# Order of the two expert products on TensorE: first product in one piece, second product whole

## The chip, the cores and the metric

The kernel runs on one core of a Trainium2 chip. The metric is the device time of one execution in microseconds (us). Its core has TensorE (PE, matmuls), VectorE (DVE), ScalarE (ACT), GpSimd (POOL), and SyncE (SP), which issues DMAs. Each engine works through its own list of instructions in order and waits on semaphores for the others.

## The reference

Three stages follow each other: an attention with a decaying state, and two mixtures of experts. Cut to the part that the change touches:

```python
def _moe_ref(x, expert_emb, tau, w1, w2):          # N = 3072 rows, D = 384, E = 8 experts, F = 1024
    ...
    expert_idx = np.argmax(logits, axis=1)
    ...
    for e in range(E):
        mask = expert_idx == e
        h = np.maximum(x[mask] @ w1[e], 0.0)
        out[mask] = gate_w[mask, None] * (h @ w2[e])

def _moe2_ref(x, w_gate, w_output_gate, w1, w2):   # x is the output of _moe_ref
    logits = x @ w_gate
    e_idx = np.argmax(logits, axis=1)
    ...
    eom = 1.0 / (1.0 + np.exp(-(x @ w_output_gate)))
    ...                                            # the same two products, with weights of its own
        out[mask] = gate_w[mask, None] * eom[mask, e, None] * ye
```

## The kernel before

After the attention the rows are sorted by expert into DRAM, in tiles of 128 rows; a tile belongs to one expert. There are two expert layers, `m = 0` and `m = 1`, and in each a loop over tiles, whose counter is `p`, runs on PE, DVE and ACT at once (27 tiles in the first layer, 28 in the second).

Every product is split in three terms, since x, h and the weights are held as a high and a low part: high times high, high times low, low times high. For a tile PE does:

- `transpose_h(p)` (L1102): eight transposes of `hs`, the hidden activations of tile p. ACT copies them from PSUM as `hT_hi` (L565), and DVE makes the rest, `hT_lo` (L875).
- `first_product(p + 1, n, ...)` (L1087, L1092): nine matmuls of 512 columns for one half n of the hidden columns of the next tile. Six read `xT_hi`, three `xT_lo`. ACT turns the result into `hs` (L560).
- the second product of tile p: 16 matmuls of 384 columns that read `hT_hi` (L1113, `second_product_hi`), and 8 that read `hT_lo` (L1121, `second_product_lo`), all into bank 2. DVE scales the sum into `ybuf` (L894, `gated`).
- `transpose_x(p + 2)` (L1076): three transposes of the tile that a DMA has brought into `xin`.

In the first layer the router of the second layer is worked in as well, on the tile whose output is just finished: `transpose_y` (L1047) transposes `ybuf`; ACT copies it to `yT` (L532); `logits_y` (L1054) multiplies it with the gates' weights; DVE picks the expert as a one-hot row (`choose`, up to L832); `ranks_y` (L1059, L1060) counts the rows ahead of each row; DVE works out the row's place (`place_row`), and GpSimd scatters the row.

Weights arrive as raw pieces, six for an expert. ACT copies each to `w_hi` (`split_hi`, L506) and DVE takes the rest, `w_lo` (`split_lo`, L735). `with_next_expert` does this in two stops of three pieces each: `SOON` in the tile that is the first of an expert, `LATE` in the tile after it, for the expert that comes next. On ACT both stand between the copies of `hT_hi` and the copy of `yT`.

The tile's weights lie in one of two slots. `weights(g)` (L1070, L1071) loads the slot and the number of the expert into registers of PE's sequencer from a table in SBUF.

Of the kernel before, what the change touches and what calls it, by code (L numbers as in the profile page):

```python
# [18 lines left out]
DM = H * D  # L19
# [8 lines left out]
JC = F // P  # L28
# [11 lines left out]
W2 = KC * F  # L40
# [22 lines left out]
def build(nc, rk_in, w_in, rkv_src, seq_in, uflat_in, emb_in, tau_in, wall1_in, wg2_in, wall2_in, out):  # L63
# [4 lines left out]
    with ExitStack() as ctx:  # L68
# [6 lines left out]
        bank = [ctx.enter_context(nc.psum_tensor(f"bank{i}", [P, 512], F32)) for i in range(8)]  # L75
# [87 lines left out]
        w_hi = sb("w_hi", [P, RING, WCOLS], F32R)  # L163
# [773 lines left out]
        def _(pe):  # L937
# [119 lines left out]
            def ranks_y(g, totals=False):  # L1057
                pe.wait_ge(r2["oh"], g)
                pe.matmul(bank[3][:, 32:32 + E], before[:, :], ohr, start=True, stop=False)  # L1059
                last = pe.matmul(bank[3][:, 32:32 + E], ones[:, :], acc, start=False, stop=True)  # L1060
                if totals:
                    pe.matmul(bank[3][:, 48:48 + E], ones[:, :], ohr, start=True, stop=False)
                    last = pe.matmul(bank[3][:, 48:48 + E], ones[:, :], acc, start=False, stop=True)
                last.then_inc(r2["cnt"], 1)

            for m in range(2):
# [35 lines left out]
                            last = pe.transpose(bank[4 + hf][:, j * P:(j + 1) * P], hs[:, n0:n0 + P], ident[:, :])  # L1102
                        last.then_inc(mo["hT_ps"], 1)

                def second_product_hi(g, slot, pieces):

                    pe.wait_ge(w_split, pieces + RAWS)
                    pe.wait_ge(mo["y_sb"], g + 1)
                    for j in range(JC):
                        if j % 4 == 0:  # L1110
                            pe.wait_ge(mo["hT_hi"], 2 * g + j // 4 + 1)
                        for w in (w_hi, w_lo):
                            pe.matmul(bank[2][:, 0:DM], hT_hi[:, j, :],  # L1113
                                      w[:, bass.ds(slot, 1), W2 + j * DM:W2 + (j + 1) * DM].rearrange("p o n -> p (o n)"),
                                      start=(j == 0 and w is w_hi), stop=False)

                def second_product_lo(g, slot):
                    for j in range(JC):
                        if j % 4 == 0:
                            pe.wait_ge(mo["hT_lo"], 2 * g + j // 4 + 1)  # L1120
                        last = pe.matmul(bank[2][:, 0:DM], hT_lo[:, j, :],  # L1121
                                         w_hi[:, bass.ds(slot, 1), W2 + j * DM:W2 + (j + 1) * DM].rearrange("p o n -> p (o n)"),
                                         start=False, stop=(j == JC - 1))
                    last.then_inc(mo["mm2"], 1)

                pe.sem_inc(mo["mm2"], 2)
# [8 lines left out]
                with pe.Fori(0, last) as p:  # L1135
                    slot, pieces = weights(p + 1)
                    transpose_h(p)
                    first_product(p + 1, 0, slot, pieces)
                    if m == 0:
                        transpose_y(p + 1)  # L1140
                    old_slot, old_pieces = weights(p)
                    second_product_hi(p, old_slot, old_pieces)
                    if m == 0:
                        logits_y(p + 1)
                    first_product(p + 1, 1, slot, pieces)
                    transpose_x(p + 2)
                    if m == 0:
                        ranks_y(p + 1)
                    second_product_lo(p, old_slot)

                transpose_h(last)
                slot, pieces = weights(last)
                if m == 0:
                    transpose_y(last + 1)
                    logits_y(last + 1)
                second_product_hi(last, slot, pieces)
                if m == 0:
                    ranks_y(last + 1)
                second_product_lo(last, slot)
                if m == 0:  # L1160
                    transpose_y(last + 2)
                    logits_y(last + 2)
# [46 lines left out]
```

## Time and profile before

| | |
|---|---|
| time, median of 3 runs | 946.95 us (946.66 to 947.95) |
| time of the profiled execution | 947.32 us |
| its span from first to last instruction | 945.6 us |
| PE busy | 775.7 us, 82% of the span |
| DVE busy | 569.5 us, 60% |
| ACT busy | 392.2 us, 41% |
| first expert layer's loop | about 335 to 640 us of the span |
| second expert layer's loop | about 669 to 934 us of the span |

The profile follows one execution. Busy time is the time in which an engine had an instruction of its own in work; PE's matmuls overlap, so that the start of one to the start of the next is their pace, not their duration.

### The profile page before, as it was taken

The numbers are of one execution on the slowest core, as the hardware profiler recorded it, in microseconds if no ns is written. First come the engines' busy times: TensorE is split into PE (matmuls) and PEld (weight loads), VectorE is DVE, ScalarE is ACT, GpSimd is POOL, SyncE is SP. The second block draws the span as 40 slices with busy tenths as digits, with TensorE's granted clock in tenths as the row PEclk, the third lists the DMA queues.
The fourth block names the chain that finished last, engine by engine and source line by source line (L and its number), as shares of the span: only waits on it lengthen the run. The fifth ranks groups of instructions, "written<-read, shape, count | busy, mean of one in ns | idle before, by whom it ended". The sixth has DMA issues, their size and how long they took to land.

```text
span 945.6 us, 20223 instructions
## 1 busy us (share of the span) xinstructions
PE 775.7 (82%) x4774; PEld 678.1 (72%) x4775; DVE 569.5 (60%) x1437; ACT 392.2 (41%) x768; POOL 196.1 (21%) x218
## 2 busy tenths in 40 slices
PE   0686877667780199999999999992999999999995
PEld 0575766556530188989888898881899999999994
DVE  4999999999364035574747556654444535434631
ACT  2344344443470034453535545530443534434531
POOL 5544444445005400000100000000001010101010
PEclk9979788897895599999999999996899999999998
DMA  4453534455174302441414335332344424333310
GB/s 110 126 138 113 148 102 138 116 145 209 35 234 169 118 17 68 132 157 50 160 43 160 100 100 165 101 100 86 101 140 142 136 71 167 109 101 104 104 37 30
DMA packets 46726, 108.30 MB, mean 115 GB/s; under 512 B 6601, under 2 KB 25616, under 8 KB 46704
## 3 DMA queue, kind: packets, MB, share of 16 engines
q1 hardware_dynamic: 29632, 67.91, 23.2%
q10 hardware_dynamic: 11952, 25.88, 9.2%
q0 software_dynamic: 5120, 14.26, 4.1%
q8 instruction: 7, 0.11, 0.1%
q14 instruction: 15, 0.12, 0.0%
HBM read 90.60 MB, written 19.01 MB: 116 GB/s over the span
## 4 chain that ended last, share of the span: by engine, by line
PE 63%; DVE 18%; issue 10%; ACT 3%; ACTq 2%; POOL 1%; SPq 1%; DMA 1%; DVEq 0%; POOLq 0%
PE bank L1087 16%; PE bank L1113 15%; PE bank L1121 8%; PE bank L1092 8%; DVE Q L643 6%; PE bank L1102 5%; DVE SF L653 4%; PE bank L1076 2%; PE bank L1054 2%; PE bank L1029 2%; ACT w_hi L506 2%; DVE Kb L657 2%; DVE St L675 1%; DVE Rq L648 1%; PE bank L1012 1%
## 5 line engine op out<-in xcount | busy, mean ns | idle before, releaser
L735 DVE TENSOR_TENSOR w_lo<-raw,w_hi 128x1024 f32 (+1 forms) x96 | 112.1, 1221 | 66.0 <-ACT w_hi L506 66.0
L1113 PE MATMUL bank<-w_hi,hT_hi 128*128 x440 | 150.3, 342 | 1.0 <-ACT hT_hi L565 0.5
L1113 PE MATMUL bank<-w_lo,hT_hi 128*128 x440 | 147.8, 336 | 0.0
L1087 PE MATMUL bank<-w_hi,xT_hi 128*128 x330 | 138.9, 421 | 1.6 <-ACT xT_hi L556 1.6
L1087 PE MATMUL bank<-w_lo,xT_hi 128*128 x330 | 131.9, 400 | 0.0
L560 ACT ACTIVATE hs<-bank 128x512 f32<-128x512 f32 x110 | 65.1, 592 | 114.1 <-PE bank L1092 106.8
L506 ACT ACTIVATE w_hi<-raw 128x1024 f32 (+1 forms) x96 | 94.8, 1049 | 38.6 <-issue 38.6
L1092 PE MATMUL bank<-w_hi,xT_lo 128*128 x330 | 95.2, 397 | 0.0
L565 ACT ACTIVATE hT_hi<-bank 128x512 fp32r<-128x512 f32 x110 | 59.7, 595 | 76.1 <-PE bank L1102 76.1
L1121 PE MATMUL bank<-w_hi,hT_lo 128*128 x440 | 90.9, 348 | 0.0
L414 POOL DMA_INDIRECT sorted<-yrow,slot x28 | 27.2, 972 | 300.8 <-DVE yrow L853 300.8
L951 PE MATMUL bank<-Rq,Kb 64*128 64x128 f32 x384 | 38.5, 358 | 61.4 <-DVE Kb L657 61.4
L1113 PEld LDWEIGHTS bank<-w_hi,hT_hi 128*128 128x128 f32 x440 | 82.6, 188 | 7.3 <-issue 6.1
L869 DVE TENSOR_TENSOR xT_lo<-bank,xT_hi 128x384 fp32r<-128x384 f32 x57 | 31.8, 558 | 92.5 <-ACT xT_hi L556 92.5
L1113 PEld LDWEIGHTS bank<-w_lo,hT_hi 128*128 128x128 f32 x440 | 82.6, 188 | 1.2
L428 POOL DMA_INDIRECT out<-ybuf,toki x28 | 27.2, 972 | 260.8 <-DVE ybuf L894 260.8
L951 PEld LDWEIGHTS bank<-Rq,Kb 64*128 64x128 f32 x384 | 32.7, 253 | 66.9 <-DVE Kb L657 60.2
L1121 PEld LDWEIGHTS bank<-w_hi,hT_lo 128*128 128x128 f32 x440 | 74.8, 189 | 0.0
L1076 PE MATMUL bank<-ident,xin 128*128 128x128 f32 x171 | 28.7, 278 | 56.1 <-DMA xin<-sorted 56.1
L1092 PEld LDWEIGHTS bank<-w_hi,xT_lo 128*128 128x128 f32 x330 | 62.8, 190 | 14.4
L1087 PEld LDWEIGHTS bank<-w_hi,xT_hi 128*128 128x128 f32 x330 | 63.6, 193 | 12.8 <-issue 2.4
L875 DVE TENSOR_TENSOR hT_lo<-bank,hT_hi 128x512 fp32r<-128x512 f32 x110 | 70.9, 686 | 2.9 <-ACT hT_hi L565 1.3
(194 smaller groups left out, 1320.8 us busy)
## 6 DMA issues: line engine op xcount, KB each, us to landing
raw<-wall_in SPq DMA_DIRECT2D x96, 512.0 KB, 3.9
rkv<-rkv_src ACTq DMA_DIRECT2D x24, 576.0 KB, 5.3
xin<-sorted ACTq DMA_DIRECT2D x59, 194.0 KB
rk<-rk_in SPq DMA_DIRECT2D x48, 192.0 KB, 3.7
wb<-w_in SPq DMA_DIRECT2D x48, 96.0 KB, 3.4
sorted<-padrow SPq DMA_DIRECT2D x16, 194.0 KB, 1.9
sorted<-yrow,slot POOLq DMA_INDIRECT x28, 2.6
out<-ybuf,toki POOLq DMA_INDIRECT x28, 2.6
```

The costliest lines, as they stand in the source:

```text
L506: act.activation(w_hi[:, slot, q * RAWC:(q + 1) * RAWC], raw[:, q], ACT.Copy).then_inc(w_his, 1)
L560: act.activation(hs[:, n * 512:n * 512 + 512], bank[n][:, :], ACT.Relu).then_inc(mo["h_sb"], 1)
L565: act.activation(hT_hi[:, 4 * n:4 * n + 4], bank[4 + n][:, :].rearrange("p (k t) -> p k t", k=4), ACT.Copy)\
L643: last = v.tensor_tensor_scan(Q[:, b, a, 1:C + 1], wb[:, par, a, 0:C], wb[:, par, a, 0:C], 1.0, ALU.mult, ALU.bypass)
L735: v.tensor_tensor(w_lo[:, slot, cols], raw[:, q], w_hi[:, slot, cols].bitcast(F32), ALU.subtract).then_inc(w_split, 1)
L875: v.tensor_tensor(hT_lo[:, 4 * n:4 * n + 4], bank[4 + n][:, :].rearrange("p (k t) -> p k t", k=4), hT_hi[:, 4 * n:4 * n + 4].bitcast(F32), ...
L951: last = pe.matmul(bank[2 * (b % 2) + hf][:, a * C:(a + 1) * C], Kb[q, b, a, :], Rq[q, b, a, :], start=True, stop=True, skip_group_check=True)
L1076: last = pe.transpose(bank[6][:, k * P:(k + 1) * P], xin[:, k * P:(k + 1) * P], ident[:, :])
L1087: pe.matmul(bank[n][:, :], xT_hi[:, k, :], w[:, bass.ds(slot, 1), cols].rearrange("p o n -> p (o n)"), start=(k == 0 and w is w_hi), stop= ...
L1092: last = pe.matmul(bank[n][:, :], xT_lo[:, k, :], w_hi[:, bass.ds(slot, 1), k * F + c0:k * F + c0 + 512].rearrange("p o n -> p (o n)"), st ...
L1113: pe.matmul(bank[2][:, 0:DM], hT_hi[:, j, :], w[:, bass.ds(slot, 1), W2 + j * DM:W2 + (j + 1) * DM].rearrange("p o n -> p (o n)"), start=( ...
L1121: last = pe.matmul(bank[2][:, 0:DM], hT_lo[:, j, :], w_hi[:, bass.ds(slot, 1), W2 + j * DM:W2 + (j + 1) * DM].rearrange("p o n -> p (o n)" ...
```

## The change

PE alone gets another order inside the loops of both expert layers, and at their ends. `first_product` for both halves now stands together, ahead of the router's logits and of the second product. The second product is one function: for each of the eight slices j, both terms of `hT_hi` and the term of `hT_lo` follow one another. Its waits for `hT_lo` stand with those for `hT_hi`. `ranks_y` is called in its middle, ahead of slice 4.

```diff
-                def second_product_hi(g, slot, pieces):
+                def second_product(g, slot, pieces, between=None):
 
                     pe.wait_ge(w_split, pieces + RAWS)
                     pe.wait_ge(mo["y_sb"], g + 1)
                     for j in range(JC):
                         if j % 4 == 0:
                             pe.wait_ge(mo["hT_hi"], 2 * g + j // 4 + 1)
-                        for w in (w_hi, w_lo):
-                            pe.matmul(bank[2][:, 0:DM], hT_hi[:, j, :],
...
-                def second_product_lo(g, slot):
-                    for j in range(JC):
-                        if j % 4 == 0:
                             pe.wait_ge(mo["hT_lo"], 2 * g + j // 4 + 1)
...
+                        if j == 4 and between is not None:
+                            between()
+                        for x, w in ((hT_hi, w_hi), (hT_hi, w_lo), (hT_lo, w_hi)):
+                            last = pe.matmul(bank[2][:, 0:DM], x[:, j, :],
+                                             w[:, bass.ds(slot, 1), W2 + j * DM:W2 + (j + 1) * DM].rearrange("p o n -> p (o n)"),
+                                             start=(j == 0 and x is hT_hi and w is w_hi), stop=(j == JC - 1 and x is hT_lo))
                     last.then_inc(mo["mm2"], 1)
...
                     if m == 0:
                         transpose_y(p + 1)
                     old_slot, old_pieces = weights(p)
-                    second_product_hi(p, old_slot, old_pieces)
+                    first_product(p + 1, 1, slot, pieces)
                     if m == 0:
                         logits_y(p + 1)
-                    first_product(p + 1, 1, slot, pieces)
                     transpose_x(p + 2)
-                    if m == 0:
-                        ranks_y(p + 1)
-                    second_product_lo(p, old_slot)
+                    second_product(p, old_slot, old_pieces, (lambda: ranks_y(p + 1)) if m == 0 else None)
```

The first place is PE in the first layer's loop, behind the loads of `weights(p)`. ISA rows are register steps of the sequencer. Before:

```order
L1047 MATMUL bank<-ident,ybuf 128x128 x3
L1070 ISA
L1070 TENSOR_LOAD tab
L1070 ISA x2
L1071 ISA
L1071 TENSOR_LOAD tab
L1071 ISA x2
L1107 ISA
L1113 ISA
L1113 MATMUL bank<-w_hi,hT_hi 128x384
```

Now, from the last of these loads on:

```order
L1071 TENSOR_LOAD tab
L1071 ISA x2
L1087 ISA
L1087 MATMUL bank<-w_hi,xT_hi 128x512
L1087 REGISTER_ALU
L1087 MATMUL bank<-w_lo,xT_hi 128x512
```

The first product's second half has taken the place of the 16 matmuls of `second_product_hi`; the register step at L1107, which belongs to a wait of the second product, has gone from here.

The second place is PE around the logits (L1054) in the same loop. Before, the 16 matmuls of L1113 stood ahead of them:

```order
L1113 MATMUL bank<-w_lo,hT_hi 128x384
L1054 MATMUL bank<-rtW,yT 128x16 x3
L1087 ISA
L1087 MATMUL bank<-w_hi,xT_hi 128x512
L1087 REGISTER_ALU
```

Now the first product's second half, 9 matmuls, stands ahead of them, and the second product starts behind the transposes of x:

```order
L1092 MATMUL bank<-w_hi,xT_lo 128x512 x3
L1054 MATMUL bank<-rtW,yT 128x16 x3
L1074 ISA
L1076 MATMUL bank<-ident,xin 128x128 x3
L1107 ISA
L1116 ISA
L1116 MATMUL bank<-w_hi,hT_hi 128x384
```

The third place is PE around the ranks (L1059, L1060) and the end of the tile. Before:

```order
L1076 MATMUL bank<-ident,xin 128x128 x3
L1059 MATMUL bank<-r,before 128x8
L1060 MATMUL bank<-r,ones 128x8
L1121 MATMUL bank<-w_hi,hT_lo 128x384 x8
L1135 REGISTER_ALU
L1135 COMPARE_AND_BRANCH
L1099 ISA
```

Now, of the four slices that follow the ranks, the first:

```order
L1116 MATMUL bank<-w_hi,hT_lo 128x384
L1059 MATMUL bank<-r,before 128x8
L1060 MATMUL bank<-r,ones 128x8
L1116 ISA
L1116 MATMUL bank<-w_hi,hT_hi 128x384
L1116 REGISTER_ALU
L1116 MATMUL bank<-w_lo,hT_hi 128x384
L1116 MATMUL bank<-w_hi,hT_lo 128x384
```

Eight matmuls without a register step between the ranks and the loop's branch have become four slices of three matmuls with two register steps each.

## Rows read from the trace of the kernel before

**Rows 1.** Busy time by stretch: span, each engine, PEclk, DMA share, GB/s.

```profile
338.00:640.00 302.00, 297.06 (x1745) 266.32 (x1743) 181.03 (x660) 143.32 (x307) 25.26 (x26) 1.00 0.33 105
672.00:930.00 258.00, 257.10 (x1424) 233.84 (x1424) 121.50 (x204) 111.53 (x177) 25.27 (x26) 1.00 0.34 111
```

**Rows 2.** Waits of PE over the span: us in total, times, longest us.

```profile
PE bank L1054 <- ACT yT L532: 4.7, 9, 1.4
```

**Rows 3.** Groups by line, ACT, 338 to 642 us: busy, mean ns, idle before.

```profile
L506 ACT ACTIVATE w_hi<-raw 128x1024 f32 x42 | 41.4, 1050 | 19.4 <-issue 19.4
```

**Rows 4.** Timeline of PE, a plain tile of layer one: start us, duration us.

```profile
482.31 1.03 PE L1102 MATMUL bank<-ident,hs 128*128 128x128 f32 x8
...
485.27 0.49 PE L1047 MATMUL bank<-ident,ybuf 128*128 128x128 f32 x3
...
485.71 0.43 PE L1113 MATMUL bank<-w_hi,hT_hi 128*128 x1
...
488.59 0.73 PE L1054 MATMUL bank<-rtW,yT 128*128 128x16 f32 x6
...
489.18 0.48 PE L1087 MATMUL bank<-w_hi,xT_hi 128*128 x1
...
491.33 0.49 PE L1076 MATMUL bank<-ident,xin 128*128 128x128 f32 x3
...
492.02 1.64 PE L1121 MATMUL bank<-w_hi,hT_lo 128*128 x8
...
493.50 0.27 PE L1102 MATMUL bank<-ident,hs 128*128 128x128 f32 x1
```

**Rows 5.** Timeline row of PE's weight loads, then lines of PE's sequencer (first, last start).

```profile
485.70 0.19 PEld L1113 LDWEIGHTS bank<-w_hi,hT_hi 128*128 128x128 f32 x1 [0.19 <-issue]
...
L1107 PEldq FUSED_REGOPS  x1: 42/42/42, 485.4 to 485.4; - x1
...
L1113 PEldq FUSED_REGOPS  x3: 46/51/65, 485.6 to 486.1; - x3
```

**Rows 6.** Timeline of ACT and PE, the first layer-one tile of an expert.

```profile
496.97 2.96 ACT L506 ACTIVATE w_hi<-raw 128x1024 f32 x3 [1.75 <-issue]
499.83 0.47 ACT L532 ACTIVATE yT<-bank 128x384 f32<-128x384 f32 x1
500.35 0.84 PE L1054 MATMUL bank<-rtW,yT 128*128 128x16 f32 x6 [0.41 <-ACT yT L532]
...
505.35 0.27 PE L1102 MATMUL bank<-ident,hs 128*128 128x128 f32 x1
```

**Rows 7.** Timeline of ACT and PE, the tile after that one.

```profile
510.94 0.47 ACT L532 ACTIVATE yT<-bank 128x384 f32<-128x384 f32 x1
511.52 0.78 PE L1054 MATMUL bank<-rtW,yT 128*128 128x16 f32 x6
...
516.50 0.27 PE L1102 MATMUL bank<-ident,hs 128*128 128x128 f32 x1
```

**Rows 8.** DVE's timeline and PE's sequencer, the tile of Rows 6.

```profile
502.56 0.29 DVE L832 TENSOR_SCALAR r<-iota,r 128x8 f32<-128x8 f32 x1
...
L1135 PEldq ALU_OP  x1: 32/32/32, 503.0 to 503.0; - x1
...
L1099 PEldq FUSED_REGOPS  x1: 42/42/42, 504.9 to 504.9; - x1
```

**Rows 9.** Chain that ended last, entry of layer two: start us, duration us.

```profile
657.48 2.38 DMA xin<-sorted
...
661.59 2.92 PE bank L1087 x6
```

**Rows 10.** Timeline of DVE and PE, last tile of layer two.

```profile
929.66 0.69 DVE L875 TENSOR_TENSOR hT_lo<-bank,hT_hi 128x512 fp32r<-128x512 f32 x1
...
929.89 0.44 PE L1113 MATMUL bank<-w_hi,hT_hi 128*128 x1 [0.46 <-ACT hT_hi L565]
```

**Rows 11.** Timeline of PE, last tile of layer one.

```profile
633.95 0.84 PE L1054 MATMUL bank<-rtW,yT 128*128 128x16 f32 x6 [1.40 <-ACT yT L532]
```

More of the change, by code:

```diff
@@ L1111, in second_product_hi @@
                             pe.wait_ge(mo["hT_hi"], 2 * g + j // 4 + 1)
-                        for w in (w_hi, w_lo):
-                            pe.matmul(bank[2][:, 0:DM], hT_hi[:, j, :],
-                                      w[:, bass.ds(slot, 1), W2 + j * DM:W2 + (j + 1) * DM].rearrange("p o n -> p (o n)"),
-                                      start=(j == 0 and w is w_hi), stop=False)
-                def second_product_lo(g, slot):
-                    for j in range(JC):
-                        if j % 4 == 0:
-                            pe.wait_ge(mo["hT_lo"], 2 * g + j // 4 + 1)
-                        last = pe.matmul(bank[2][:, 0:DM], hT_lo[:, j, :],
-                                         w_hi[:, bass.ds(slot, 1), W2 + j * DM:W2 + (j + 1) * DM].rearrange("p o n -> p (o n)"),
-                                         start=False, stop=(j == JC - 1))
+                            pe.wait_ge(mo["hT_lo"], 2 * g + j // 4 + 1)
+                        if j == 4 and between is not None:
[4 more added lines that the diff above has]
+                                             start=(j == 0 and x is hT_hi and w is w_hi), stop=(j == JC - 1 and x is hT_lo))
                     last.then_inc(mo["mm2"], 1)
@@ L1155, in _ @@
                     logits_y(last + 1)
[L1156 to L1159, printed above, removed]
+                second_product(last, slot, pieces, (lambda: ranks_y(last + 1)) if m == 0 else None)
                 if m == 0:
```

## The prediction

> **What bounds the kernel now.** I read the busy time by stretch first. In both expert loops PE is busy nearly throughout: 297.06 of 302 us in the first layer, 257.10 of 258 us in the second, at a granted clock of 1.00 [rows 1]. So both loops go at PE's pace, and there are only two things that an order can change: the time in which PE stands, and nothing else, since the matmuls stay the same in number and size. The second layer leaves 0.9 us of standing in 258; it has nothing to gain. Next I read PE's waits: in the first layer it waits for one thing, the copy of yT by ACT ahead of the logits, 4.7 us in 9 waits [rows 2]. The timeline shows when. A plain tile takes 493.50 - 482.31 = 11.19 us [rows 4], and the logits find yT ready. In the first tile of an expert ACT first splits three pieces of weights, from 496.97 for 2.96 us, and the copy of yT ends at 499.83 + 0.47 = 500.30; the logits start at 500.35, with PE idle, and the tile takes 505.35 - 493.50 = 11.85 us [rows 4, 6]. In the tile after it the next three pieces are split; yT is ready at 511.41, the logits start at 511.52, and the tile takes 11.15 us: there the copy comes just in time [rows 6, 7]. The 42 splits of the first layer are 14 such stops of three [rows 3], 7 of each kind, in 26 tiles of the loop; 12 tiles are plain.
>
> A smaller loss stands behind the transposes of y: PE's weight load is idle for 0.19 us because the sequencer only then gets through the register loads and the waits of the second product [rows 5].
>
> **The change, part by part.** Offsets are from a tile's first transpose of h.
>
> *The logits are reached earlier.* Between the transposes of y and the logits stood 16 matmuls, 488.59 - 485.71 = 2.88 us. Now 9 matmuls of the first product stand there, 491.33 - 489.18 = 2.15 us [rows 4]. So PE is at the logits 0.73 us earlier, while nothing on ACT's way to yT has moved: transposes of h, two copies, the splits, the copy. In a plain tile that is harmless. In a tile with splits PE cannot go past the logits, and what was covered is now a wait. Behind the logits there now stands 2.88 us of work instead of 2.15.
>
> First tile of an expert: the logits stay at 500.35, and the 5.00 us from there to the next tile [rows 6] become 5.73. Cost 0.73 us, 7 times: 5.1 us.
>
> The tile after it: the logits could start 0.05 us behind yT, as in the other tile, so at 511.46 instead of 511.52; from there 4.98 us [rows 7] become 5.71. Cost 0.67 us, 7 times: 4.7 us.
>
> *The transposes of y are followed by the first product.* The register step of the second product's waits at 485.4 and the first of its matmuls' register steps at 485.6 lie 0.2 us apart, and then the matmuls start, at 485.71 [rows 4, 5]. The first product's second half has none of these waits, so the sequencer is there 0.2 us sooner and the gap of 0.19 us should all but close. In the 14 tiles with splits this gains nothing, since they are held by yT. In the 12 plain tiles I take 0.17 us: -2.0 us; bounds 0 and -0.19 x 12 = -2.3.
>
> *The ranks stand in the middle.* PE's sequencer stops at the ranks until DVE has the one-hot row, at 502.85 in the tile shown. From there it needs 0.15 us to the branch at 503.0, with the ranks and all eight low terms dispatched on the way, and 1.9 us more for the branch and the next tile's register loads, to 504.9; the next tile's transposes start at 505.35 [rows 4, 6, 8]. That leaves 0.45 us. In the new order four slices with two register steps each stand between ranks and branch. Such slices follow each other by 0.25 us [rows 5], so 1.0 us is added, while the tile's end moves by only 0.73. What is left is 0.18 us, and from the register step at L1107 to the matmul it took 0.3 [rows 4, 5]. So the transposes come late by about 0.1 us in each of the 14 tiles: +1.5 us. Bounds: 0, and 0.3 x 14 = +4.2. In plain tiles the one-hot row is early with the logits, and nothing is late.
>
> *The low parts are wanted earlier.* In the loop DVE has made hT_lo long before: the second product now starts after the whole first product. The cover is missing only in the last tile of the second layer, where there is no first product: PE started at 929.89, behind ACT's copy; the first half of hT_lo is there only at 929.66 + 0.69 = 930.35 [rows 10]. If PE follows 0.05 us behind, as at the logits, the cost is 0.5 us; 0.2 us more for a longer hand-over would make it 0.7. I take 0.6 us, once. In the last tile of the first layer the wait for yT, 1.40 us, covers it [rows 11].
>
> *The transposes of x move some 3 us forward,* ahead of the second product. The transfer takes 2.38 us [rows 9] and is issued by ACT before its first copy of the tile, so it lands by about 3 us into the tile, and the transposes come no sooner than at 5. Hidden. The relu of the second half, the copies of xT and DVE's place_row come earlier too; all of them were covered.
>
> *The pace of the merged product.* The 16 high terms take 0.18 us each with their start, 8 low terms 493.50 - 492.02 = 1.48 us, 0.185 each with theirs [rows 4]. The starts are as many as before. I take the same pace; 0.002 us either way on 440 low terms is 1 us.
>
> **Sum:** 5.1 + 4.7 - 2.0 + 1.5 + 0.6 = +9.9 us. Against the profiled execution, 947.32 us, that is 957.2; the median of the runs is 0.37 us lower, so 956.9. Forecast: 957 us, 1.1% more.
>
> **The rivals.**
>
> *Faster.* The gap behind the transposes of y closes in all 26 tiles and the logits wait no longer than before: -0.19 x 26 + 0.6 = -4.3 us, 942.6 against the median. It decides if ACT has yT within 5.4 us of the tile's start in the tiles with splits as well. The rows have it at 6.80 and 6.06 [rows 4, 6, 7], and nothing on ACT is moved. 3 in 100.
>
> *No change.* The merged product, three terms of one slice in a row, runs at a quicker pace: 0.165 us instead of 0.174 on 1320 matmuls would be -12 us, and the total about 945 to 947. High and low terms keep the same pace now, whatever reads what [rows 4]. 4 in 100.
>
> *The sequencer is late in every tile.* If the four slices behind the ranks cost their 1.0 us also where I count room, 0.3 us in the 12 plain tiles and 0.5 in the 14: +3.6 + 7 on 9.8 + 0.6, about 968. The room in a plain tile speaks against it. 6 in 100.
>
> *The clock falls.* The waits for yT grow from 0.6 to about 1.3 us and double in number. If after each of the 14 PE ran one second product at the lower level, 1.2 GHz, at which six matmuls of the first product took 2.92 us [rows 9], against 0.23 us each now, that is some 4 us each: +56 us, 1013. Against it: a wait of 1.40 us stands in the stretch whose granted clock is 1.00, the 2.4 GHz level [rows 1, 11]. 3 in 100.
> The Trainium skill has a rule for this, "TensorE: Matmul & The Clock Gate", section "A second HAM failure mode: psum-queue depth-cycling": frequent short idle times between groups of matmuls can make the clock swing between its two levels. By that rule the sum would be the 1013 us of this rival; by the trace it stays at 957.
>
> **How the numbers follow.** The forecast's mechanism has the remaining 84 in 100. Its own range: without the sequencer's loss, with the whole gap gained and a quicker pace, 957.0 - 1.5 - 0.3 - 1 = 954.2; with the sequencer's upper bound, half the gap gained and a slower pace, 957.0 + 2.7 + 1 + 1 = 961.7. I give 953.5 to 961.5. A measurement of this kernel tells about 0.2%, 1.9 us, from no change. Faster: 0.03. Within it: 0.04. Slower: 0.93.
>
> **What would show it.** PE's wait for yT at the logits should grow from 4.7 us in 9 waits to about 14 us in 16. The first tile of an expert should take about 12.6 to 12.7 us, the next 11.9, a plain one 11.0, and a tile of the second layer should keep its pace. The idle 0.19 us of the weight load behind the transposes of y should vanish. In the last tile PE should wait for hT_lo. The forecast is wrong if yT is ready earlier in the tiles with splits, if a plain tile grows (the sequencer), or if the granted clock in the loops leaves 1.00.

## The result, and the profile after

The changed kernel takes 961.88 us (median of 4 runs, 961.0 to 963.24), the kernel before 946.86 us beside it (4 runs). The ratio is 1.0157, 95% interval 1.014 to 1.0175: slower, as forecast, and 0.4 us above the upper end of the range. The profiled execution took 963.24 us, 15.92 more than that of before; its span, 961.5 us, is longer by the same 15.9.

I read PE's waits first, over the span: what PE waited for, us in total, times, longest.

```profile
PE bank L1054 <- ACT yT L532: 15.4, 16, 1.4
...
PE bank L1116 <- DVE hT_lo L875: 1.2, 1, 1.2
```

The wait for yT went from 4.7 us in 9 [rows 2] to 15.4 in 16, and in the last tile the low parts are waited for: both were forecast. What was not forecast is in the busy time by stretch. Columns as in [rows 1]; the first two rows are the loops, the other six divide one first tile of an expert, 404.61 to 418.70. The last three figures are the granted clock, the DMA share and GB/s.

```profile
338.00:640.00 302.00, 288.57 (x1665) 261.19 (x1664) 174.49 (x619) 136.85 (x297) 24.29 (x25) 0.97 0.32 104
690.00:940.00 250.00, 249.93 (x1388) 227.26 (x1388) 118.23 (x199) 107.56 (x174) 25.27 (x26) 1.00 0.35 114
404.60:407.00 2.40, 2.40 (x16) 2.12 (x15) 1.91 (x5) 1.09 (x2) 0.97 (x1) 1.00 0.22 83
407.00:409.90 2.90, 2.90 (x16) 2.23 (x14) 0.66 (x2) 1.81 (x2) 0.00 (x0) 1.00 0.00 0
409.90:412.40 2.50, 1.19 (x10) 0.93 (x9) 2.50 (x3) 2.41 (x5) 0.00 (x0) 1.00 0.29 84
412.40:414.00 1.60, 1.60 (x9) 1.60 (x8) 1.46 (x7) 0.00 (x0) 0.00 (x0) 0.63 0.87 310
414.00:416.00 2.00, 2.00 (x8) 2.00 (x7) 0.35 (x4) 1.35 (x5) 0.00 (x0) 0.50 0.87 291
416.00:418.60 2.60, 2.60 (x17) 2.60 (x17) 1.55 (x9) 0.00 (x0) 0.00 (x0) 0.95 0.51 187
```

The granted clock of the first loop is 0.97, where it was 1.00 [rows 1]. Inside the tile it is 1.00 up to 412.40, falls to 0.50 (1.2 GHz, the lower of its two levels) behind a stretch in which PE was busy for 1.19 of 2.50 us, and is back before the tile ends. The second loop keeps 1.00.

The timeline of PE shows what each kind of tile became. First the end of a first tile of an expert that kept its clock, then the tile after it, then a plain tile (start us, duration us, idle before):

```profile
376.09 0.84 PE L1054 MATMUL bank<-rtW,yT 128*128 128x16 f32 x6 [1.30 <-ACT yT L532]
...
381.62 0.34 PE L1116 MATMUL bank<-w_hi,hT_lo 128*128 x1
381.80 0.61 PE L1102 MATMUL bank<-ident,hs 128*128 128x128 f32 x4
...
387.93 0.84 PE L1054 MATMUL bank<-rtW,yT 128*128 128x16 f32 x6 [0.61 <-ACT yT L532]
...
393.65 1.04 PE L1102 MATMUL bank<-ident,hs 128*128 128x128 f32 x8
...
396.61 0.49 PE L1047 MATMUL bank<-ident,ybuf 128*128 128x128 f32 x3
396.85 0.48 PE L1087 MATMUL bank<-w_hi,xT_hi 128*128 x1
...
399.01 0.73 PE L1054 MATMUL bank<-rtW,yT 128*128 128x16 f32 x6
```

Behind the first tile's last matmul at 381.62 the next transposes start 0.18 us later: the sequencer isn't late. The tile after it runs from 381.80 to 393.65, 11.85 us, with a wait of 0.61 us for yT. The plain tile ends at 404.61, where the next fence begins, after 10.96 us; the first product follows the transposes of y with no gap, and the logits find yT ready. Now the tile of the windows above:

```profile
404.61 1.04 PE L1102 MATMUL bank<-ident,hs 128*128 128x128 f32 x8
...
409.29 0.86 PE L1092 MATMUL bank<-w_hi,xT_lo 128*128 x3
411.47 0.84 PE L1054 MATMUL bank<-rtW,yT 128*128 128x16 f32 x6 [1.31 <-ACT yT L532]
412.16 0.52 PE L1076 MATMUL bank<-ident,xin 128*128 128x128 f32 x3
412.44 0.42 PE L1116 MATMUL bank<-w_hi,hT_hi 128*128 x1
...
412.88 0.52 PE L1116 MATMUL bank<-w_hi,hT_lo 128*128 x1
413.20 0.52 PE L1116 MATMUL bank<-w_hi,hT_hi 128*128 x1
...
416.96 0.34 PE L1116 MATMUL bank<-w_hi,hT_lo 128*128 x1
...
418.70 0.27 PE L1102 MATMUL bank<-ident,hs 128*128 128x128 f32 x1
```

The wait is the same, 1.31 us, and yT is as early. But from 412.88 on ten matmuls start 0.32 us apart instead of 0.17, and the tile takes 14.09 us. That is 10 x 0.15 = 1.5 us lost in a single tile.

The lengths of all tiles, worked out from the starts of the first transpose of h (L1102):

```
us per tile               before          after
12 plain tiles            11.20 (mean)    10.99
7 first of an expert      11.87           12.58 in two; 14.08 to 14.14 in five
7 after them              11.20           11.84
second layer, usual       9.58            9.53 (up to 9.93 in four)
last tile to the end      17.21           17.92
```

The first loop is 310.44 instead of 295.93 us long: 7 x 0.71 = 5.0 and 7 x 0.64 = 4.5 for the waits, 5 x 1.52 = 7.6 for the clock, 12 x -0.21 = -2.5 for the plain tiles; together 14.6 (14.5 by the loop's own length, the rest is rounding). The second loop takes 0.8 us less, the tail 0.7 more, the stretch between the loops 0.15 more. The 1.4 us by which the first loop starts later (336.12, before 334.76) belong to no edit: over the kernels below, which have the same work ahead of it, that start lies anywhere from 331.5 to 337.9. The five parts add up to the 15.9 us. The other three runs of the changed kernel left no trace, so in how many of their tiles the clock fell isn't known.

### The profile page after: what moved, and what is told of

Same layout as the page of the kernel before. It is cut to its first block, busy times and chain, and to the rows that moved or that the text cites. A ratio compares the mean times of both kernels' runs of the same rounds, so it can differ in the third digit from the quotient of the medians.

```text
span 961.5 us, 20305 instructions
## 1 busy us (share of the span) xinstructions
PE 773.9 (80%) x4774; PEld 679.3 (71%) x4775; DVE 568.1 (59%) x1437; ACT 388.3 (40%) x768; POOL 197.3 (21%) x218
## 4 chain that ended last, share of the span: by engine, by line
PE 57%; DVE 16%; issue 10%; ACT 4%; POOL 4%; ACTq 3%; DMA 2%; SPq 1%; DVEq 0%; POOLq 0%
PE bank L1116 25%; PE bank L1087 12%; PE bank L1092 6%; DVE Q L643 5%; PE bank L1102 4%; DVE SF L653 3%; ACT w_hi L506 2%; PE bank L1076 2%; PE bank L1054 2%; POOL sorted L403 2%; PE bank L1029 2%; DVE Kb L657 2%; ACTq L239 1%; DMA xin<-sorted 1%; PE bank L1012 1%
## 5 line engine op out<-in xcount | busy, mean ns | idle before, releaser
L1116 PE MATMUL bank<-w_hi,hT_hi 128*128 x440 | 158.4, 360 | 1.2 <-DVE hT_lo L875 1.2
L1116 PE MATMUL bank<-w_lo,hT_hi 128*128 x440 | 151.9, 345 | 0.0
L1116 PE MATMUL bank<-w_hi,hT_lo 128*128 x440 | 151.7, 345 | 0.0
L1116 PEld LDWEIGHTS bank<-w_hi,hT_hi 128*128 128x128 f32 x440 | 85.4, 194 | 1.7 <-issue 1.4
L1116 PEld LDWEIGHTS bank<-w_hi,hT_lo 128*128 128x128 f32 x440 | 85.6, 195 | 0.0
L1116 PEld LDWEIGHTS bank<-w_lo,hT_hi 128*128 128x128 f32 x440 | 85.5, 194 | 0.0
L560 ACT ACTIVATE hs<-bank 128x512 f32<-128x512 f32 x110 | 63.0, 586 | 50.1 <-PE bank L1092 50.1
L1087 PEld LDWEIGHTS bank<-w_lo,xT_hi 128*128 128x128 f32 x330 | 63.5, 192 | 11.1
```

The costliest lines, as they stand in the source:

```text
L560: act.activation(hs[:, n * 512:n * 512 + 512], bank[n][:, :], ACT.Relu).then_inc(mo["h_sb"], 1)
L1087: pe.matmul(bank[n][:, :], xT_hi[:, k, :], w[:, bass.ds(slot, 1), cols].rearrange("p o n -> p (o n)"), start=(k == 0 and w is w_hi), stop= ...
L1116: last = pe.matmul(bank[2][:, 0:DM], x[:, j, :], w[:, bass.ds(slot, 1), W2 + j * DM:W2 + (j + 1) * DM].rearrange("p o n -> p (o n)"), star ...
```

## The experiments

**The order alone.** The kernel before, with the next tile's second half of the first product moved; the three terms of the second product stay apart.

```diff
-                    second_product_hi(p, old_slot, old_pieces)
+                    first_product(p + 1, 1, slot, pieces)
                     if m == 0:
                         logits_y(p + 1)
-                    first_product(p + 1, 1, slot, pieces)
                     transpose_x(p + 2)
+                    second_product_hi(p, old_slot, old_pieces)
                     if m == 0:
                         ranks_y(p + 1)
                     second_product_lo(p, old_slot)
```

> The kernel before with only the first product's second half moved ahead of the logits and of the high terms; high and low terms stay apart, with the ranks between them. Theory: the early logits alone make the wait for yT and the fall of the granted clock, so the time is about that of the changed kernel, 960 to 963 us; the first tile of an expert takes 12.6 us, or 14.1 where the clock falls. Rival, that the merged product or the ranks in its middle bring the fall: 952 to 955 us, no tile of 14.1 us.

It took 962.0 us (one run; 946.34 before). Tile by tile it is the changed kernel: 10.99, 12.57, 11.83 us, and 14.07 to 14.14 in the same five first tiles of an expert. One of those on PE's timeline:

```profile
410.84 0.84 PE L1054 MATMUL bank<-rtW,yT 128*128 128x16 f32 x6 [1.29 <-ACT yT L532]
...
412.24 0.51 PE L1113 MATMUL bank<-w_hi,hT_hi 128*128 x1
412.54 0.53 PE L1113 MATMUL bank<-w_lo,hT_hi 128*128 x1
```

A tile of the second layer takes 9.53 us, as in the changed kernel. So, as far as one run tells, the whole effect is the order's, the 0.05 us gained in the second layer too. Merging the terms and placing the ranks in their middle cost nothing here.

**The merging alone.** The second product with its three terms together, in its old place: five slices, logits, first product, transposes of x, ranks, three slices.

```diff
-                    second_product_hi(p, old_slot, old_pieces)
+                    second_product(p, old_slot, old_pieces, rng=range(0, 5))
...
-                    second_product_lo(p, old_slot)
+                    second_product(p, old_slot, old_pieces, rng=range(5, JC))
```

> The kernel before with the three terms merged but in the old place: slices 0 to 4 of the second product (15 matmuls) ahead of the logits, then the first product's second half, the transposes of x, the ranks, and slices 5 to 7. Theory: the logits find yT as before, no fall of the clock, so within 2 us of the kernel before; if the register steps behind the ranks hold the sequencer, the first tile of an expert is 0.3 us longer, 2 us in all. Rival, that merging costs by itself: 953 us or more.

955.22 us (953.48 to 958.78), ratio 1.0105, interval 1.0076 to 1.0134. I had expected no more than 2 us; the time is where the rival of the expectation had it. The clock is 1.00, so the loss is another one. Three slices are 9 matmuls where 8 stood; that is 0.17 us behind the wait. And the sequencer is late. The register step ahead of the transposes, by line and engine (first and last start), for the end of a first tile of an expert:

```profile
L1099 PEldq FUSED_REGOPS  x1: 42/42/42, 416.0 to 416.0; - x1
```

And the same place on PE's timeline:

```profile
415.86 0.34 PE L1119 MATMUL bank<-w_hi,hT_lo 128*128 x1
416.14 0.65 PE L1102 MATMUL bank<-ident,hs 128*128 128x128 f32 x4
```

The step comes at 416.0, behind the last matmul's start, and the transposes start 0.28 us behind that matmul instead of 0.17. First tiles of an expert take 12.28 to 12.40 us, those after them 11.62 to 11.80, plain ones 11.22 in the mean (before: 11.20). In the tiles after them 0.13 of the 0.52 us lost lies ahead of the logits, which start 6.40 us into the tile instead of 6.27 (means), and 0.39 behind them, 5.32 instead of 4.93: the ninth matmul's 0.17, and in the tile that ends at 427.89 another 0.16 between the last matmul and the transposes (0.33 us instead of 0.17). The late sequencer that I had feared for the changed kernel is real, but shows where PE waits less for yT.

**The transposes of x ahead of the logits**, in the changed kernel. PE then stands 0.3 us less in a tile with splits.

```diff
                     first_product(p + 1, 1, slot, pieces)
+                    transpose_x(p + 2)
                     if m == 0:
                         logits_y(p + 1)
-                    transpose_x(p + 2)
```

> The changed kernel with the transposes of x ahead of the logits instead of behind them. The wait for yT is 0.33 us shorter in 14 tiles: -4.6 us. Theory that the length of the wait in which PE stands decides on the clock: from 1.4 to 1.1 us standing, fewer or no falls, down to 950 us. Rival, that the whole stretch without long matmuls decides, 2.5 us before and 2.2 now: falls stay, 955 to 958 us.

958.01 us (957.85 to 958.94), ratio 1.013, interval 1.0113 to 1.0146. The clock falls in no tile of the loop. The busy time of the first loop:

```profile
338.00:640.00 302.00, 290.86 (x1706) 260.51 (x1705) 176.34 (x638) 138.09 (x301) 24.93 (x26) 1.00 0.32 104
```

And a first tile of an expert on PE's timeline:

```profile
410.17 0.84 PE L1054 MATMUL bank<-rtW,yT 128*128 128x16 f32 x6 [1.00 <-ACT yT L532]
...
415.42 0.34 PE L1116 MATMUL bank<-w_hi,hT_lo 128*128 x1
415.84 1.09 PE L1102 MATMUL bank<-ident,hs 128*128 128x128 f32 x8
```

The wait is 1.00 us instead of 1.30 and the clock stays. But the tile shortens only to 12.53, not to 12.28: 0.42 us pass between the last matmul and the transposes, a quarter of a microsecond more than its pace. Here the sequencer is the bound, as the step of the forecast on the ranks had it. The tiles after them take 11.87 to 12.12: longer than in the changed kernel, since ACT's splits begin 0.30 us later in them (3.05 us into the tile). Why they do isn't shown.

**PE kept busy while it would stand.** The changed kernel with eight matmuls of 384 columns to an unused place ahead of the logits, in every tile of the first layer. What they compute is read by nothing.

```diff
+                        for k in range(8):
+                            pe.matmul(bank[3][:, 128:512], xT_hi[:, k % 3, :],
+                                      w_hi[:, bass.ds(slot, 1), (k % 3) * F:(k % 3) * F + 384].rearrange("p o n -> p (o n)"),
+                                      start=True, stop=True, skip_group_check=True)
                         logits_y(p + 1)
```

> The changed kernel with 8 extra matmuls of 384 columns ahead of the logits in the first layer's loop; they go to an unused part of bank 3 and nothing reads them. They fill the wait in the first tile of an expert, 8 x 0.174 = 1.4 us. Theory, that standing makes the clock fall: granted clock 1.00 in the loop, first tile of an expert 12.6 to 12.7 us in all seven; plain tiles and second tiles at about 12.4 us, so the whole at about 975 us. Rival, that the fall has another cause: tiles of 14.1 us remain, 983 us.

975.4 us (one run). All seven first tiles take 12.57 to 12.60 us, all others of the loop 12.37 to 12.58. In the stretch 338 to 640 us:

```profile
338.00:640.00 302.00, 302.00 (x1794) 278.77 (x1793) 167.67 (x595) 131.60 (x283) 23.33 (x24) 1.00 0.30 98
```

With 1.4 us more work in them (PE stood for 1.3) the five fallen tiles are 1.5 us shorter. The fillers are all that was added, so the fall needs PE's standing; the rest of the tile's rows doesn't bring it about by itself.

**How long it must stand.** The same with two such matmuls, 0.33 us: PE waits as long as with the transposes of x first, but these stay behind the logits.

> The changed kernel with two matmuls of 384 columns to an unused place ahead of the logits in every tile of the first layer (they compute nothing that is used), 0.33 us of PE. In the first tile of an expert PE then stands 1.1 us instead of 1.45, as long as in the kernel with the transposes of x ahead of the logits, but the transposes stay behind the logits. Theory that the length of the standing makes the clock fall: no tile falls, the seven first tiles take 12.58, the plain and the others grow by 0.2 to 0.33, the total is 961.9 - 7.6 + 12 x 0.33 + 7 x 0 = about 958. Rival, that the row of short matmuls behind the wait (logits and transposes of x, nine in all) makes it fall: five tiles still take 14.1, the total about 966.

958.19 us (one run; 947.31 before). First tiles 12.55 to 12.58, those after them 11.82 to 11.87, plain ones 11.33. The loop's busy time:

```profile
338.00:640.00 302.00, 293.38 (x1743) 266.32 (x1742) 175.85 (x635) 137.32 (x299) 24.30 (x25) 1.00 0.32 104
```

And one of its waits on PE's timeline:

```profile
410.23 0.84 PE L1054 MATMUL bank<-rtW,yT 128*128 128x16 f32 x6 [0.97 <-ACT yT L532]
```

In the first tiles of an expert a wait of 0.97 us is never followed by a fall here, one of 1.30 us in the changed kernel is in five of seven. The rival, that the short matmuls behind the wait are enough by themselves, is out: they stand here as they did there. (This holds for these tiles. In the last tile of the layer, outside the loop, PE waits 1.41 us, and the clock falls there in this kernel too.) A third of a microsecond of useless work makes the kernel some 4 us faster (958.2 against 961.9, each beside about 947 of before).

**A longer stop in the old order.** The kernel before with the logits ahead of the second half of the high terms, so that PE stands longer than in the changed kernel (`between` is `logits_y`).

```diff
                     for j in range(JC):
                         if j % 4 == 0:
                             pe.wait_ge(mo["hT_hi"], 2 * g + j // 4 + 1)
+                        if j == 4 and between is not None:
+                            between()
```

> The kernel before with the logits ahead of slice 4 of the high terms, so behind 8 of them instead of 16; nothing else is moved. They are reached 1.4 us earlier. Theory that standing makes the clock fall, now without the new order: the first tile of an expert stands for about 2.0 us and its clock falls in most of the 7, 13.3 us + 1.5 us = 14.8 us; the tile after stands for 1.2 us, less than the 1.4 us at which it fell, and takes 12.4 us; plain tiles keep 11.2 us. In all about 975 us. Rival, that the fall belongs to the new order: 965 us, granted clock 1.00.

971.64 us (one run). The clock falls here too, so it needs no new order, and it falls less often than I expected: two of seven first tiles (14.85 and 14.89 us, the others 13.29 to 13.32) and the two tiles behind those (14.13 and 14.12, with waits of 1.21 and 1.24 us; the others 12.56 to 12.59, with 1.04 to 1.14). The profile puts these waits down to `issue`, but the logits start as soon as ACT has copied yT (456.95 + 0.47 = 457.42, logits at 457.52). Two first tiles, the one that kept its clock and the one that didn't:

```profile
409.12 0.81 PE L1054 MATMUL bank<-rtW,yT 128*128 128x16 f32 x6 [1.82 <-issue]
415.54 0.71 PE L1102 MATMUL bank<-ident,hs 128*128 128x128 f32 x5
...
457.52 0.81 PE L1054 MATMUL bank<-rtW,yT 128*128 128x16 f32 x6 [1.82 <-issue]
465.48 0.71 PE L1102 MATMUL bank<-ident,hs 128*128 128x128 f32 x5
```

The same wait, 1.82 us, and from the logits to the next tile 6.42 us in one, 7.96 in the other. So the length of the wait alone doesn't say whether the clock falls.

**The logits inside the second product**, ahead of its third slice; the ranks ahead of the seventh. It is meant to give the changed kernel its cover back.

```diff
                     first_product(p + 1, 1, slot, pieces)
                     transpose_x(p + 2)
-                    second_product(p, old_slot, old_pieces, (lambda: ranks_y(p + 1)) if m == 0 else None)
+                    second_product(p, old_slot, old_pieces,
+                                   at={2: lambda: logits_y(p + 1), 6: lambda: ranks_y(p + 1)} if m == 0 else {})
```

> The changed kernel with the logits moved into the second product, ahead of slice 2, and the ranks ahead of slice 6. The logits then come at 6.8 us into a tile, when yT is there: no wait worth naming, clock 1.00. But the sequencer gets from the one-hot row to the next tile's transposes in 0.15 + 0.5 (two slices) + 1.9 us, which is late: plain tiles 11.4 us, first tiles of an expert 12.0, in all 952 to 956 us. Rival, that the sequencer has room: 11.0 and 11.2 us, about 942 us.

953.45 us (one run). No fall; first tiles 12.0 to 12.1, those after them 11.3 to 11.5, plain ones 11.23 to 11.29 (but 11.47 in the loop's first and 11.08 in its last). The waits for yT are gone from PE's list in that loop, and the sequencer's have come in their place. PE's waits, 336 to 630 us:

```profile
PE bank L1102 <- issue: 4.9, 12, 0.6
```

The next transposes wait for nothing that the profile shows but PE's own sequencer. So this place of the logits gives the cover back and loses most of it to the sequencer: 8 us faster than the changed kernel, still some 7 slower than before. Other places at this end weren't tried.

**The register loads moved.** The kernel before, with the loads for the next tile behind the transposes of h, those for the old tile ahead of the transposes of y, in both layers.

```diff
-                    slot, pieces = weights(p + 1)
                     transpose_h(p)
+                    slot, pieces = weights(p + 1)
                     first_product(p + 1, 0, slot, pieces)
+                    old_slot, old_pieces = weights(p)
                     if m == 0:
                         transpose_y(p + 1)
-                    old_slot, old_pieces = weights(p)
```

> The kernel before with the table loads moved on PE alone: those for the next tile behind the transposes of h, those for the old slot ahead of the transposes of y. The gap of 0.2 us behind the transposes of y closes; that helps only the 12 plain tiles, since the others are held by yT: 944.5 us, -2.4 us. Rival, that the loads only shift the gap to another place: no change.

969.88 us (968.43 to 972.72), ratio 1.0238, interval 1.0217 to 1.0259. In the first layer it did what was expected (plain tiles 11.0, the others as before). In the second each tile takes 10.44 us instead of 9.58, 0.86 more on 27 tiles: 23 us. PE's timeline there:

```profile
713.55 1.04 PE L1102 MATMUL bank<-ident,hs 128*128 128x128 f32 x8
714.68 0.49 PE L1087 MATMUL bank<-w_hi,xT_hi 128*128 x1
...
716.16 0.86 PE L1092 MATMUL bank<-w_hi,xT_lo 128*128 x3
717.28 0.44 PE L1113 MATMUL bank<-w_hi,hT_hi 128*128 x1 [0.26 <-issue]
```

From the transposes of h to the first product it takes 1.13 us (in the kernel before 0.80, in the second layer's tile that starts at 736.79), and in front of the second product PE stands again. It is the first load's move that costs this: with the second alone moved, below, the second layer keeps 9.58 us. The sequencer used to do the loads while PE worked off what was queued ahead of the transposes. In this tile the last step of them comes only at 714.3, and the first product starts at 714.68. In the first layer the same loads cost nothing, the first product follows the transposes by 0.79 us: there they begin 1.35 us ahead of the transposes (493.2, 494.55), in the second layer 0.9 us ahead (723.1, 723.99). Why the two layers differ isn't shown further.

**The same, with the logits between the high and the low terms of the first product's second half**, and the ranks ahead of the last four low terms.

> The run with moved table loads, and the logits between the high and the low terms of the first product's second half (behind 22 matmuls and so at about 7.35 us into a tile, past yT's 6.8), the ranks ahead of the last four low terms. No wait for yT, no sequencer late: 11.0 us in all 26 tiles, 936 to 938 us. Rival, that the late ranks make DVE and the sequencer late: 11.3 us or more in tiles with splits, 943 us or more.

978.69 us (977.73 to 980.53), ratio 1.0342, interval 1.032 to 1.0365. Every tile of the first layer but the loop's first takes 11.68 to 11.92, also the plain ones; a tile of the second 10.2. PE's waits, 340 to 640 us:

```profile
PE bank L1087 <- issue: 7.4, 25, 0.4
```

The first product behind the transposes waits for the sequencer in 25 tiles. The moved loads alone don't do that: in the kernel above they cost the first layer nothing (plain tiles 11.0 us). What is new here is the late logits and ranks, as the rival of the expectation had it; by how much each of them counts isn't told. The logits start 8.28 us into the tile at 405.32, not at 7.35. That a tile of the second layer takes 10.2 us and not 10.44, in the same order, isn't explained either.

**Only the second load moved**, from the kernel before.

```diff
                     first_product(p + 1, 0, slot, pieces)
+                    old_slot, old_pieces = weights(p)
                     if m == 0:
                         transpose_y(p + 1)
-                    old_slot, old_pieces = weights(p)
```

> The kernel before with one edit in both layers: the register loads of the old tile's slot and pieces stand ahead of the transposes of y, so the sequencer does them while PE is still busy with the first product; the other loads stay where they are. Theory of the sequencer: the gap of 0.19 us behind the transposes of y closes in the plain tiles, which go from 11.19 to about 11.0 us, nothing changes in the tiles with splits (they are held by yT) or in the second layer; 12 x -0.19 = -2.3, so 944.6 (range 943.5 to 945.8). Rival: the gap belongs to the waits and not to the loads, then 946.9.

945.53 us (10 runs, 943.23 to 947.81; 21 runs of before in the same series, 947.32), ratio 0.9977, interval 0.9962 to 0.9992. The plain tiles take 11.00 us, the second layer 9.58. That is the gap of [rows 5], gained without moving the logits. Either is enough to close it: here the waits of the second product still stand there and the loads are gone, in the changed kernel the loads stand there and the waits are gone.

**And the second layer in the new order**, the first layer in the old.

```diff
+                    if m == 1:
+                        first_product(p + 1, 1, slot, pieces)
+                        transpose_x(p + 2)
                     second_product_hi(p, old_slot, old_pieces)
                     if m == 0:
                         logits_y(p + 1)
-                    first_product(p + 1, 1, slot, pieces)
-                    transpose_x(p + 2)
-                    if m == 0:
+                        first_product(p + 1, 1, slot, pieces)
+                        transpose_x(p + 2)
                         ranks_y(p + 1)
```

> As the run before it, and in the second layer alone the first product stands in one piece ahead of the second (terms apart as before). The clock cannot fall there, since nothing waits for yT. By the traces of the changed order a tile of the second layer goes from 9.58 to about 9.53 us, 24 times, less up to 0.7 us where the transposes of x now wait for their transfer: 943.3 to 944.3. Rival: the pace of the second layer comes from the merging and not from the order, then as the run before it.

943.37 us (10 runs, 942.49 to 945.41), ratio 0.9972, interval 0.9955 to 0.9989. A tile of the second layer takes 9.53 us, save one of 10.34, one of 9.79 and two of 9.58 and 9.62, where the transposes of x come later. These take back nearly all of the 24 x 0.05 = 1.2 us. What the order adds to the kernel above isn't told apart by the ratios.

**And the transposes of x ahead of the logits in the old order.**

```diff
                     if m == 0:
+                        transpose_x(p + 2)
                         logits_y(p + 1)
                         first_product(p + 1, 1, slot, pieces)
-                        transpose_x(p + 2)
                         ranks_y(p + 1)
```

> As the run before it, and in the first layer the transposes of x stand ahead of the logits, so 0.3 us of work lies ahead of the logits and not behind them. Where PE waits for yT the tile should shorten by 0.3 us: 7 first tiles of an expert from 11.87 to about 11.57, 7 tiles after them from 11.20 to about 11.0: -3.3 us, so about 940.5. Rival: the sequencer cannot be back from the one-hot row in less time, 11.75 in the first tiles: 942.5. Rival on the other side: the transposes of x wait for their transfer, which makes it no faster than the run before it.

941.1 us (6 runs, 938.95 to 942.66), ratio 0.9935, interval 0.9912 to 0.9957: the fastest kernel of this study. A first tile of an expert:

```profile
407.64 0.49 PE L1076 MATMUL bank<-ident,xin 128*128 128x128 f32 x3
...
408.44 0.84 PE L1054 MATMUL bank<-rtW,yT 128*128 128x16 f32 x6 [0.32 <-ACT yT L532]
...
413.14 1.03 PE L1102 MATMUL bank<-ident,hs 128*128 128x128 f32 x8
```

From the logits to the next tile it is 4.70 us instead of 5.00 [rows 6], and the tile takes 11.54. It is the reverse of the change in question: more cover ahead of the wait for yT, less work behind it. The 0.9935 is for all three edits together: the second load, the second layer's order and this one.

## Why the prediction was off

**The two waits for yT** were right in place, number and size: 0.71 us in each first tile of an expert against a forecast of 0.73, 0.64 in each tile after it against 0.67. **The gap behind the transposes of y** closed in the plain tiles, 0.21 us each against 0.17. **The pace of the merged product** is unchanged. **The last tile** waits for hT_lo and is 0.71 us longer, against 0.6.

**The step that failed is the last rival, "The clock falls".** I had the waits grow from 0.6 us, while a first tile of an expert showed 0.41 [rows 6]; they grew to 1.3. I gave it 3 in 100, priced it for all 14 tiles or none, at 4 us each, and left it out of the sum because one wait of 1.40 us had gone by at a granted clock of 1.00 [rows 1, 11]. It falls in five of the seven first tiles and costs 1.52 us in each, 7.6 us in all. Without it the changed kernel would stand at 961.9 - 7.6 = 954.3, inside the range (by the profiled execution, the only one whose tiles are known, 963.2 - 7.6 = 955.6). The measurements on which this rests: kept busy, the same tiles don't fall; with 0.33 us less standing they don't either; with the order changed and nothing else they do.

The evidence against it was luck. The wait of [rows 11] is one wait, the only one of its length. The changed kernel has the same wait in the same place, 1.40 us ahead of the logits of the first layer's last tile, and there the clock did fall. First the kernel before, then the changed one, in the same columns as above:

```profile
634.50:637.00 2.50, 2.50 (x17) 2.50 (x17) 1.22 (x8) 0.64 (x4) 0.00 (x0) 1.00 0.01 3
```

```profile
650.00:652.50 2.50, 2.50 (x16) 2.50 (x17) 1.23 (x8) 0.67 (x4) 0.00 (x0) 0.85 0.02 7
652.50:656.00 3.50, 3.50 (x16) 3.50 (x16) 1.05 (x8) 0.00 (x0) 0.00 (x0) 0.62 0.00 0
```

Nor does it take the new order. The kernel with only the second load moved has the kernel before's own last tile, instruction for instruction, with the same wait, and the clock falls in it:

```profile
634.56 0.84 PE L1054 MATMUL bank<-rtW,yT 128*128 128x16 f32 x6 [1.40 <-ACT yT L532]
```

```profile
637.60:640.60 3.00, 3.00 (x15) 3.00 (x14) 0.34 (x4) 0.00 (x0) 0.00 (x0) 0.65 0.00 0
```

Of the 14 traces of this study, that of before among them, eleven have a wait of 1.40 or 1.41 us there, and the clock falls behind it in nine, all but the kernel before and the one with eight fillers. Nothing is seen of these falls in the time: from this tile's start to the second loop's it takes 38.17 us before, 38.19 with the fall shown. Whether a wait of this length is followed by a fall varies, so one that wasn't says little of seven more. The size was wrong as well: I took a whole second product at the lower level, and it was ten of its 24 matmuls.
The Trainium skill, "TensorE: Matmul & The Clock Gate", section "A second HAM failure mode: psum-queue depth-cycling", says that frequent short idle times between groups of matmuls can make the clock swing; on the direction this case's trace agrees (0.97 in the loop, 0.50 inside a tile).

**The sequencer** was put at +1.5 us and cost nothing: behind the ranks the transposes follow at the pace of the matmuls, 0.18 us. It has no room to spare, though. Where PE waits 0.3 us less, or the logits come later, the sequencer ends the tile, and both repairs of the new order, transposes of x first and logits inside, end at 958.0 and 953.5 us. With the transposes of x first, where the sequencer is the bound, it is 3.17 us from the end of the one-hot row (412.67) to the next transposes (415.84). The changed kernel has 3.22 for it (378.58 to 381.80), so 0.05 us to spare. My terms add up to 0.15 + 1.0 + 1.9 + 0.3 = 3.35 us, 0.2 too many.

**The transposes of x are not always hidden.** Four tiles of the second layer are 0.03 to 0.40 us longer, 0.7 us together: PE now reaches the transposes 5.0 us into the tile (7.8 before), and the transfer isn't always there. The longest of the four, by the waits of 723.6 to 733 us and by what the trace has on xin:

```profile
PEld bank L1076 <- DMA xin<-sorted: 0.5, 1, 0.5
```

```profile
DMA to landing us min/median/max: 6.1/6.1/6.1
```

In the round of the loop before it the same transfer took 2.3 us, which I had taken for all. **A tile of the second layer** is otherwise 0.05 us shorter, 1.2 us in all, and the loop's first tile 0.3; I had them unchanged. With the 0.7 us back the second loop is 0.8 us shorter.

**What stays open:** which of the waits of 1.3 us and more are followed by a fall. Five of seven fall after 1.30 us, the same five in two kernels, and two of seven after 1.82. In one last tile of the first layer, that of the kernel with the logits in the first product, it fell behind two waits of 0.74 and 0.94 us. The length of the wait alone doesn't decide it, and the stretch ahead of it (the same matmuls in the tile that fell and in the one that didn't) doesn't either. The DMA traffic doesn't: in the first 1.6 us of the second product its share is 0.87 in the tile that fell (412.40 to 414.00) and 0.87 in one that kept its clock (377.00 to 378.60), and in the fallen last tiles above it is 0.00 to 0.02.

## What to carry to other kernels

When an order moves a wait forward on the engine that is the bound, the loss is the cover taken away, per tile, and it can be read to a few hundredths of a microsecond from two rows; but on TensorE add to it what the clock may take where the wait grows, as here from 1.00 to 1.30 us, and don't rule that out by a single wait that went well: look at the same place in several traces. Ask in the same breath where PE's sequencer stands: its loads, moved to a place with too little queued ahead of them, cost 0.86 us a tile here, as much as five matmuls. What helped here is work moved from behind a late wait to in front of it (11.87 to 11.54 us in a first tile of an expert), not the other way.

## What was not expected of the hardware

- The granted clock fell to 0.50 some 1.4 us after PE had resumed work, not while it stood: in the tile shown the logits start at 411.47 and the first slow matmul at 412.88.
- The transfer of xin, 2.3 us from issue to landing in one tile of the second layer, took 6.1 us in the next.
- In the first tiles of an expert waits of 0.96 to 1.02 us brought no fall in fourteen, waits of 1.28 to 1.36 us did in ten of fourteen, waits of 1.79 to 1.83 us in two of seven.
- In the last tile of the first layer the same wait of 1.40 or 1.41 us was followed by a fall in nine of eleven traces, two of 0.74 and 0.94 us in one.
- The register loads of PE's sequencer, which cost nothing where matmuls are queued ahead of them, showed as 0.86 us in every tile of the second layer where they stand behind the transposes of h.
